# Top-k in attention: two score tiles of a pair in turn on VectorE, and the steps of three other engines laid out anew around them

## What is computed

```python
# attention: q, k, v of shape (4, 8, 576, 64)
scores = scale * np.matmul(q, k.transpose(0, 1, 3, 2))
kth = np.partition(scores, -32, axis=-1)[..., -32:-31]
scores = np.where(scores >= kth, scores, -1000000000.0)
attn = np.exp(scores - np.max(scores, axis=-1, keepdims=True))
attn = attn / (np.sum(attn, axis=-1, keepdims=True) + 1e-09)
x = np.matmul(attn, v)            # then laid out as (2304, 512)
# dense: w_in (512, 2048), w_out (2048, 512)
h = x @ w_in
x = (h * np.cos(h)) @ w_out
# experts: w_gate, w_output_gate (512, 8), w1 (8, 512, 1024), w2 (8, 1024, 512)
e = argmax(x @ w_gate)
out = softmax(x @ w_gate)[e] * sigmoid(x @ w_output_gate)[e] * (relu(x @ w1[e]) @ w2[e])
```

## Time and profile before

| what | us |
|---|---|
| median of 3 runs | 1418.0 |
| lowest and highest run | 1417.39, 1425.48 |
| profiled execution, from outside | 1417.38 |
| its span | 1415.8 |
| TensorE busy (PE) | 1266.2 (89%) |
| weight loads (PEld) | 803.3 (57%) |
| VectorE busy (DVE) | 939.5 (66%) |
| ScalarE busy (ACT) | 656.0 (46%) |
| GpSimd busy (POOL) | 562.1 (40%) |

### The profile page before, as it was taken

How to read it: one execution, slowest core, us unless ns; L and a number is a source line. 1 busy time by engine, 2 the same in 40 slices (tenths; PEclk the granted TensorE clock), 3 DMA queues, 4 the chain that set the end, 5 groups by cost and what they waited for, 6 DMA issues and landing times. The chain is left out here.

```text
span 1415.8 us, 18220 instructions
## 1 busy us (share of the span) xinstructions
PE 1266.2 (89%) x5962; PEld 803.3 (57%) x5963; DVE 939.5 (66%) x1690; ACT 656.0 (46%) x1082; POOL 562.1 (40%) x696
## 2 busy tenths in 40 slices
PE   4557899989999999899899999899399999999996
PEld 2435656856747747648658558476244444444443
DVE  6999998999999999999999999905211111111110
ACT  3455665666666766665766756624011111111110
POOL 2444463364563564654454554614411111111111
PEclk9567999999999999999999999999699999999999
DMA  8301001101001100100010000003034442243000
GB/s 245 95 8 25 1 8 33 42 8 40 1 9 41 41 8 16 25 8 16 19 47 16 1 16 1 1 16 127 24 136 150 147 150 103 73 167 128 15 13 1
DMA packets 81839, 71.52 MB, mean 51 GB/s; under 512 B 62266, under 2 KB 62266, under 8 KB 81248
## 3 DMA queue, kind: packets, MB, share of 16 engines
q1 hardware_dynamic: 76192, 60.86, 13.4%
q0 software_dynamic: 5568, 9.65, 2.2%
HBM read 62.97 MB, written 11.45 MB: 53 GB/s over the span
## 5 line engine op out<-in xcount | busy, mean ns | idle before, releaser
L720 DVE MAX8 tops<-scores_left 128x8 f32<-128x576 f32 x432 | 327.3, 758 | 12.3
L407 POOL TENSOR_TENSOR probs<-scores,probs 128x576 f32<-128x576 f32 x144 | 211.0, 1465 | 244.1 <-ACT probs L514 244.1
L976 PE MATMUL dense_banks<-x_T,weights 128*128 128x256 f32 x1024 | 246.4, 396 | 16.6 <-ACT h_T L552 16.6
L986 PE MATMUL dense_banks<-weights,h_T 128*128 128x512 f32 x512 | 236.6, 605 | 0.0
L976 PEld LDWEIGHTS dense_banks<-x_T,weights 128*128 128x128 f32 x1024 | 196.6, 197 | 58.0 <-ACT h_T L552 20.0
L723 DVE MATCH_REPLACE8 scores_left<-tops,scores_left 128x576 f32<-128x576 f32 x288 | 213.9, 743 | 0.0
L1128 PE MATMUL dense_banks<-weights,expert_h_T 128*128 x400 | 183.8, 592 | 0.0
L1109 PE MATMUL score_banks<-weights,x_gathered_T 128*128 x400 | 182.1, 598 | 1.0 <-DVE x_gathered_T L864 1.0
L514 ACT ACTIVATE probs<-scores,top_consts 128x576 f32<-128x576 f32 x144 | 111.5, 775 | 120.9 <-POOL top_consts L404 120.7
L986 PEld LDWEIGHTS dense_banks<-weights,h_T 128*128 128x128 f32 x512 | 93.4, 193 | 106.9 <-issue 106.9
L869 DVE COPY expert_h_T<-dense_banks 128x512 f32<-128x512 f32 x25 | 17.3, 692 | 185.5 <-PE dense_banks L1119 185.5
(11 more groups left out here) (160 smaller groups left out, 1581.3 us busy)
## 6 DMA issues: line engine op xcount, KB each, us to landing
weights<-in_moe_w SPq DMA_DIRECT2D x16, 2048.0 KB, 10.8
y_rows<-y_rows_sb SPq DMA_DIRECT2D x18, 256.0 KB, 2.0
k_rows<-in_k SPq DMA_DIRECT2D x32, 128.0 KB, 2.7
q_rows<-in_q SPq DMA_DIRECT2D x16, 256.0 KB, 3.4
v_rows<-in_v SPq DMA_DIRECT2D x32, 128.0 KB, 2.3
weights<-in_moe_w_in SPq DMA_DIRECT2D x1, 4096.0 KB, 13.0
weights<-in_moe_w_out SPq DMA_DIRECT2D x1, 4096.0 KB, 22.4
k_rows<-in_k SPq DMA_DIRECT2D x16, 32.0 KB, 2.6
```

The lines of the kernel that those rows point to most:

```text
L407: nc.gpsimd.tensor_tensor(ex, SS[:, u % 3, i, :], ex, ALU.subtract).then_inc(s["masked_done"], 1)
L720: V.max(top, src).then_inc(s["tops_done"], 1)
L976: last = MM(HO[:, f % 2, 0:BT], win[:, kd, f * P:(f + 1) * P], XT[:, m % 2, kd, :], start=kd == 0, stop=kd == KD - 1)
L986: last = MM(HO[:, t, :], HS[:, f, t * P:(t + 1) * P], wout[:, f, :], start=f == 0, stop=f == NF - 1)
```

## The change

On VectorE the two tiles of a pair take turns: first MAX8 of tile 0, first MAX8 of tile 1, first replacement of tile 0, and so on, seven operations each. WK has a buffer for each tile. An operation waits for the previous one of its own tile, by the count of tops_done that tops_at gives. VectorE now takes pair st in step st; the order of its pairs stays the same. The reciprocals of pair st - 2 stand behind the third operation, and the two parts of reduce_h behind the second and the third.

On GpSimd one instruction makes the constants of both tiles; a step is: constants of st - 1, denominators of st - 2, both masks of st - 1, the two products with the reciprocals for st - 2, and then all four pieces of the gate. On ScalarE a step is: copy_scores(st), both exps of st - 2, two copies of h, both below of st - 1, copy_probs(st - 3), both parts of the sine, two copies of h, copy_y, copy_x, the small copies, absolute. In TensorE's outputs the wait is for two f instead of four.

```diff
--- before.py
+++ after.py
@@ -122,6 +122,11 @@
 SMALL = small_bank_order()
 N_SMALL = len(SMALL)
 MOE_FILLS = NF + BLOCK
+
+
+def tops_at(u, i, op):
+
+    return 14 * u + 2 * op + i + 1
 
 
 def y_fill(t):
@@ -208,7 +213,7 @@
         VE = sb("v_rows", [P, HP, KB, 2 * D], stack=att)
         VR = sb("v_left", [P, HP, 2 * D], stack=att)
         SS = sb("scores", [P, 3, 2, S], stack=att)
-        WK = sb("scores_left", [P, S], stack=att)
+        WK = sb("scores_left", [P, 2, S], stack=att)
         TOP = sb("tops", [P, 3, 2, TOPK], stack=att)
         TC = sb("top_consts", [P, 3, 2, 2], stack=att)
         EX = sb("probs", [P, 3, 2 * S], stack=att)
@@ -396,15 +401,28 @@
             pool.wait_ge(s["const_ready"], n_const[0])
             pool.dma_start(table.rearrange("(p s) w -> p s w", p=P), table_init[:]).then_inc(s["table_written"], 16)
 
+            def consts(u):
+                pool.wait_ge(s["tops_done"], tops_at(u, 1, 6))
+                at_least(pool, s["exps_done"], 2 * (u - 2))
+                nc.gpsimd.tensor_tensor(TC[:, u % 3, :, :], TOP[:, u % 3, :, 0:TOPK:TOPK - 1],
+                                        factors[:].unsqueeze(1).to_broadcast([P, 2, 2]), ALU.mult).then_inc(s["consts_done"], 1)
+
             def mask(u, i):
 
-                a = u % 3
-                pool.wait_ge(s["tops_done"], (2 * u + i) * 7 + 7)
-                at_least(pool, s["exps_done"], 2 * (u - 3) + i + 1)
-                nc.gpsimd.tensor_tensor(TC[:, a, i, :], TOP[:, a, i, 0:TOPK:TOPK - 1], factors[:], ALU.mult).then_inc(s["consts_done"], 1)
                 pool.wait_ge(s["below_done"], 2 * u + i + 1)
-                ex = EX[:, a, i * S:(i + 1) * S]
+                ex = EX[:, u % 3, i * S:(i + 1) * S]
                 nc.gpsimd.tensor_tensor(ex, SS[:, u % 3, i, :], ex, ALU.subtract).then_inc(s["masked_done"], 1)
+
+            def denominators(u):
+                pool.wait_ge(s["exps_done"], 2 * u + 2)
+                at_least(pool, s["rden_done"], u - 1)
+                nc.gpsimd.tensor_scalar_add(DEN2[:, u % 2, :], DEN[:, u % 3, :], 1e-9).then_inc(s["den_done"], 1)
+
+            def normalise(u):
+                pool.wait_ge(s["rden_done"], u + 1)
+                for i in range(2):
+                    nc.gpsimd.tensor_scalar(EX[:, u % 3, i * S:(i + 1) * S], EX[:, u % 3, i * S:(i + 1) * S], RD[:, u % 2, i:i + 1], 1.0,
+                                            ALU.mult, ALU.mult).then_inc(s["probs_ready"], 1)
 
             def gate(st, piece):
 
@@ -417,24 +435,17 @@
                                                 ALU.mult).then_inc(s["gated_done"], 1)
 
             for st in range(LOOP):
-                u = st - 2
-                if 0 <= u < NS:
-                    mask(u, 1)
-                gate(st, 0)
-                if 0 <= u < NS:
-                    pool.wait_ge(s["exps_done"], 2 * u + 2)
-                    at_least(pool, s["rden_done"], u - 1)
-                    nc.gpsimd.tensor_scalar_add(DEN2[:, u % 2, :], DEN[:, u % 3, :], 1e-9).then_inc(s["den_done"], 1)
-                gate(st, 1)
+                if 0 <= st - 1 < NS:
+                    consts(st - 1)
+                if 0 <= st - 2 < NS:
+                    denominators(st - 2)
                 if 0 <= st - 1 < NS:
                     mask(st - 1, 0)
-                gate(st, 2)
-                if 0 <= u < NS:
-                    pool.wait_ge(s["rden_done"], u + 1)
-                    for i in range(2):
-                        nc.gpsimd.tensor_scalar(EX[:, u % 3, i * S:(i + 1) * S], EX[:, u % 3, i * S:(i + 1) * S], RD[:, u % 2, i:i + 1], 1.0,
-                                                ALU.mult, ALU.mult).then_inc(s["probs_ready"], 1)
-                gate(st, 3)
+                    mask(st - 1, 1)
+                if 0 <= st - 2 < NS:
+                    normalise(st - 2)
+                for piece in range(4):
+                    gate(st, piece)
 
             for t in LAST:
                 for f in range(0, NF, 4):
@@ -509,7 +520,7 @@
 
             def below(u, i):
                 a = u % 3
-                act.wait_ge(s["consts_done"], 2 * u + i + 1)
+                act.wait_ge(s["consts_done"], u + 1)
                 at_least(act, s["probsT_done"], u - 2)
                 nc.scalar.activation(EX[:, a, i * S:(i + 1) * S], SS[:, u % 3, i, :], ACT.Relu, bias=TC[:, a, i, 1:2],
                                      scale=-BIG).then_inc(s["below_done"], 1)
@@ -611,14 +622,10 @@
             for st in range(LOOP):
                 u = st - LAG
                 dense = block_at(st)
-                if 0 <= st - 2 < NS:
-                    below(st - 2, 1)
                 if st < NS:
                     copy_scores(st)
-                for m, i in dense:
-                    if i in (3, 5):
-                        sine(m, (i - 3) // 2, 1)
                 if 0 <= st - 2 < NS:
+                    exps(st - 2, 0)
                     exps(st - 2, 1)
                 for m, i in dense:
                     if i < 4:
@@ -626,16 +633,15 @@
                         copy_h(m, 4 * i + 1)
                 if 0 <= st - 1 < NS:
                     below(st - 1, 0)
+                    below(st - 1, 1)
                 if 0 <= u < NS:
                     copy_probs(u)
-                if 0 <= st - 1 < NS:
-                    exps(st - 1, 0)
                 for m, i in dense:
+                    if i in (3, 5):
+                        for h in range(2):
+                            sine(m, (i - 3) // 2, h)
                     if i < 4:
                         copy_h(m, 4 * i + 2)
-                    if i in (2, 4):
-                        absolute(m, (i - 2) // 2)
-                    if i < 4:
                         copy_h(m, 4 * i + 3)
                     if i in (6, 7):
                         copy_y(2 * m + i - 6)
@@ -655,7 +661,7 @@
                     copy_keys(b, p)
                 for m, i in dense:
                     if i in (2, 4):
-                        sine(m, (i - 2) // 2, 0)
+                        absolute(m, (i - 2) // 2)
                 if st >= LOOP - 2:
                     late_copy(LAST[0], st - (LOOP - 2))
 
@@ -707,48 +713,49 @@
         def _(dve):
             V = nc.vector
 
-            def top_k(u, i):
-                done = (2 * u + i) * 7
-                src = SS[:, u % 3, i, :]
-                if i == 0:
-                    dve.wait_ge(s["scores_copied"], u + 1)
-                at_least(dve, s["consts_done"], 2 * (u - 3) + i + 1)
-                for rnd in range(TOPK // 8):
-                    if i == 1 and rnd == 2 and u >= 1:
-                        reciprocals(u - 1)
-                    top = TOP[:, u % 3, i, rnd * 8:rnd * 8 + 8]
+            def top_op(u, i, op):
+
+                rnd = op // 2
+                top = TOP[:, u % 3, i, rnd * 8:rnd * 8 + 8]
+                src = SS[:, u % 3, i, :] if op < 2 else WK[:, i, :]
+                if op == 0:
+                    if i == 0:
+                        dve.wait_ge(s["scores_copied"], u + 1)
+                    at_least(dve, s["consts_done"], u - 2)
+                else:
+                    dve.wait_ge(s["tops_done"], tops_at(u, i, op - 1))
+                if op % 2 == 0:
                     V.max(top, src).then_inc(s["tops_done"], 1)
-                    dve.wait_ge(s["tops_done"], done + 2 * rnd + 1)
-                    if rnd < TOPK // 8 - 1:
-                        V.match_replace(WK[:], top, src, NEG).then_inc(s["tops_done"], 1)
-                        dve.wait_ge(s["tops_done"], done + 2 * rnd + 2)
-                        src = WK[:]
+                else:
+                    V.match_replace(WK[:, i, :], top, src, NEG).then_inc(s["tops_done"], 1)
 
             def reciprocals(u):
                 dve.wait_ge(s["den_done"], u + 1)
                 at_least(dve, s["probs_ready"], 2 * (u - 1))
                 V.reciprocal(RD[:, u % 2, :], DEN2[:, u % 2, :]).then_inc(s["rden_done"], 1)
 
-            def reduce_h(m, g):
-                dve.wait_ge(s["dense_emptied"], m * MOE_FILLS + 8 * (g + 1))
-                at_least(dve, s["gated_done"], (2 * (m - 1) + g + 1) * 4)
+            def reduce_h(m, g, part):
                 hs = HS[:, g * 8:(g + 1) * 8, :].rearrange("p a n -> p (a n)")
                 r1 = R[:, g, :, :].rearrange("p a n -> p (a n)")
-                V.tensor_scalar(r1.bitcast(I32), hs, 1.0 / TWO_PI, None, ALU.mult).then_inc(s["reduced_done"], 1)
-                dve.wait_ge(s["reduced_done"], m * 4 + 2 * g + 1)
-                V.scalar_tensor_tensor(out=r1, in0=r1.bitcast(I32), scalar=-TWO_PI, in1=hs,
-                                       op0=ALU.mult, op1=ALU.add).then_inc(s["reduced_done"], 1)
+                if part == 0:
+                    dve.wait_ge(s["dense_emptied"], m * MOE_FILLS + 8 * (g + 1))
+                    at_least(dve, s["gated_done"], (2 * (m - 1) + g + 1) * 4)
```

(26 more changed lines are left out.)

## The result

| what | before | after |
|---|---|---|
| median, us | 1419.31 | 1360.65 |
| lowest and highest run, us | 1417.39, 1425.48 | 1359.01, 1361.44 |
| span of the profiled execution, us | 1415.8 | 1358.9 |
| VectorE busy, us | 939.5 | 851.5 |
| TensorE busy, us | 1266.2 | 1245.0 |

The ratio is 0.9579, with an interval of 0.9556 to 0.9602: 58.7 us faster. The prediction was 1363 us.

What follows compares the result with a forecast made beforehand. VectorE was taken to set the pace, with TensorE close behind. Gains of 11 us in the first pairs, 40 in the dense steps and 3 at the end made 54, from 1417.4 to 1363 us; range 1332 to 1404.

Steps and rivals of the forecast that it cites:

- The early start: On VectorE, an instruction not held by the one in front starts 0.12 us earlier, 1.65 us a pair, giving 9.9 us.
- The first part: First ten pairs, before dense work, where VectorE alone counts: step 11 starts at about 117.4 us, 11 us gained.
- the hand-over: A pair's way through four engines, put at 9 to 10 us in the first ten steps; decides from 9.9 us on.
- The dense steps: Step 11 to the loop's end: TensorE takes over as the bound, 776 us becomes 736, 40 us gained.
- floor: TensorE's least time for the dense steps, between 700 and 723 us, taken as 711.
- pauses: TensorE's stalls and waits for h and GpSimd's products, with the clock behind them: 3.3 us a block, 25 us in all.
- rival D: TensorE's pauses vanish and the floor is reached: 91 us gained, 1326 us; chance 0.09.
- The end: Step 72: the values' 3.83 us wait for the probabilities' copy shrinks, 3 us gained; what follows is unchanged.
- A: No earlier start behind a MAX8, VectorE stays the bound at 11.56 us a pair: 1422 us; chance 0.12.
- B: Slower: the loop through four engines becomes the bound, 1479 us, or about 1435 in some steps only; chance 0.08.
- C: TensorE's pauses are worse than counted, 6 us a block instead of 3.3: 1384 us; chance 0.13.

Runs made afterwards that it cites:

- e1: Changed kernel, but VectorE sorts tile 0 to the end and then tile 1, the rest of the new plan kept: 1406.14 us, 0.9956 of the kernel before.
- e2: Changed kernel with tiles in turn, but every VectorE operation waits for the one directly in front: 1428.95 us, 1.0109 of the kernel before.
- a0: The changed kernel itself once more, nothing altered: 1358.99 us, 0.9574 of the kernel before.
- e4: Changed kernel with one search round less on VectorE (24th largest value as limit, so another result): 1320.19 us, 0.9342 of the kernel before.
- e8: Changed kernel with the reciprocals behind the second part of the reduction of h instead of in front: 1345.57 us, 0.9519 of the kernel before.
- e9: Changed kernel with two GpSimd products ahead of the normalisations and the reciprocals behind the reduction's second part: 1346.25 us, 0.9482 of the kernel before.
- e10: Kernel before with turns and two scores_left buffers, reciprocals behind the sixth operation of the pair after next: 1405.09 us, 0.9887 of the kernel before.
- e11: Changed kernel with each tile's constants in an instruction of its own, below waiting for its tile alone: 1359.25 us, 0.9568 of the kernel before.
- e3: Kernel before with only the turns and two scores_left buffers, reciprocals behind twelve operations of the next pair: 1411.08 us, 0.9991 of the kernel before.
- e6: Changed kernel with the sines back at their old places on ScalarE: 1414.24 us, 1.0007 of the kernel before.
- e5: Changed kernel with TensorE's outputs waiting for the gated pieces of four f at once, as before: 1363.27 us, 0.9651 of the kernel before.
- e7: Changed kernel with two of GpSimd's four products in front of the two normalisations: 1347.67 us, 0.9542 of the kernel before.

## Why the prediction was right, term by term

TensorE's and VectorE's rows of the changed kernel, both ends of the dense steps, against the earlier trace rows:

```profile
98.36 2.29 PE L933 MATMUL score_banks<-k_T,q_T 64*128 64x288 f32 x8
...
108.36 2.29 PE L933 MATMUL score_banks<-k_T,q_T 64*128 64x288 f32 x8
...
119.40 2.19 PE L933 MATMUL score_banks<-k_T,q_T 64*128 64x288 f32 x8
...
843.95 3.70 PE L994 MATMUL dense_banks<-weights,h_T 128*128 128x512 f32 x8
...
853.75 0.49 PE L969 MATMUL small_banks<-probs_T,v_left 128*128 128x128 f32 x2 [1.69 <-ACT probs_T L547]
...
857.61 5.90 PE L994 MATMUL dense_banks<-weights,h_T 128*128 128x512 f32 x8 [2.34 <-POOL h_T L434]
...
869.10 1.16 PE L1037 MATMUL score_banks<-x_T,weights 128*128 128x128 f32 x8
```

**The early start** was put at 0.12 us, with 0.13 as a bound. It is 0.13 to 0.14: a pair takes 9.7 us, not 9.9.

The Trainium skill ("VectorE: DVE Perf Modes", "The DRAIN you can't avoid") says that a chain of eight copies was no faster with one semaphore than with eight; the MAX8 of e1 and e2 do not agree, 0.67 to 0.68 us without the wait for the instruction in front and 0.80 with it. The same section of the Trainium skill also says that a next operation that is not held starts earlier; the prediction left that out, and with it e1 and e2 agree.

**The first part**, predicted 11 us: step 11 starts at 119.40 instead of 128.68, 9.3 us. From the seventh pair on the hand-over was the limit, as these rows of TensorE (98.36, 108.36) and this one of VectorE say:

```profile
101.85 1.42 DVE L728 MAX8 tops<-scores 128x8 f32<-128x576 f32 x2 [0.20 <-ACT scores L539]
```

The prediction had the loop at "9 to 10" in the slow clock and the decision at 9.9, and let VectorE win. It was 10.0. In a0, where the loop did not bind, step 11 starts at 116.89, 0.5 us from the predicted 117.4.

**The dense steps**, predicted 40 us: from 119.40 to 843.95 it is 724.5 us instead of 776.2, 51.6 us gained. Busy times of this stretch, before and after:

```profile
128.68:904.85 776.17, 724.33 (x4013) 508.92 (x4012) 735.28 (x1310) 512.63 (x856) 402.11 (x485) 0.97 0.08 19
```

```profile
119.40:843.95 724.55, 701.08 (x4013) 497.69 (x4012) 659.33 (x1306) 501.20 (x855) 395.70 (x425) 1.00 0.08 21
```

The same 4013 MATMULs are busy 23 us less, at the full clock, and TensorE's idle time falls from 51.8 to 23.5 us. The prediction had 711 us of floor, the middle of 700 to 723 for want of a view of how much time the slow clock took, and 25 us of pauses. With the busy time as the floor, the mis-sized term is the floor, 10 us too high, and the pauses were 1.5 too large. Measured by e4, which still has 7.1 us of waits of its own in its 705.1, the miss is 6 us of floor and 6 of pauses (19.4). The clock came back whole (0.97 to 1.00), where the twelve pauses for the products last 1.6 us at most. So rival D, which counted with the floor and no pauses, was half true.

Inside the pauses one term was too small as well: the reduction was put at 1.3 and 2.6 us, as in the earlier trace rows, and takes 1.6 and 2.9 on average, 3.48 for the second part in each block's first half, because of GpSimd beside it (e8).

**The end**, predicted 3 us: 904.85 - 843.95 = 60.9 us ahead at step 72, 63.0 at the values (853.75), so 2.1 of the 3. Then the outputs of step 73 wait 2.34 us for the products and run in slow clock (5.90 us), and at the first late tile it is 60.1 (929.22 against 869.10). That pause was not in the sum at this place. Behind it the changed kernel loses another 3 us before the routing, in two waits of ScalarE whose releaser lies outside the engines of the core; TensorE waits 7.2 us there, 4.3 in the kernel before. The same 7.2 us stand in a0, e9, e10 and e11, and 0.7 in all of e1 to e8, so they go with the chip and not with the change: e10 has the old plan and has them too. What is waited for stays open.

Together 9.3 + 51.6 - 0.8 - 3.2 = 56.9 us in the profiled executions. The total was right to 3 us because one term was 12 us too small and the three others together 9 us too large (the first part by 2, the end by 4, and 3 behind it, put at nothing). The mechanism was right; that the sum came so close is partly luck.

**Rivals.** A fell with e1 and e2. B as a whole fell, but it ruled from the seventh pair to step 11, and e3, e6 and e10, with the same early starts and 46 to 60 us slower than the changed kernel, suggest how near it was behind that. C was put at 6 us a block; the 23.5 us of idle time are 3.1 us a block.

## What to carry to other kernels

When one engine runs a chain of short operations, put another chain's operation between each two: a start is early when the thing waited for is not the instruction directly in front, and at 576 elements that is 0.13 us of 0.8. Before counting on it, lay out the whole round that the engine hands to the others and gets back, because the gain ends where that round is longer than the engine's new period; here turns without the new plan brought nothing, or 16 us at best, and the plan without the turns 6 us at best. Then look at what the release of one engine lets start on another: moving a 0.15 us reciprocal behind a reduction gave 6 to 8 us. And slack at the start of an engine's round is not slack at its end: follow the result onward, too, before calling the engine's time free.

## What the hardware showed that was not expected

GpSimd and VectorE slow each other, and not evenly. Where GpSimd's two normalisations run beside the second part of VectorE's reduction, they take 3.42 to 3.51 us instead of 1.46; the reduction takes 3.48 us instead of 2.27 in the first half of each block (149.11) and stays at 2.27 to 2.40 in the second (174.11). In e8 it is GpSimd's two masks that run beside it: they take 5.17 us instead of 2.79 (145.37), and the reduction stays at 2.27 (147.00). Which of them loses was not looked into further.

In the first ten steps the clock moves between its two levels in some executions (scores in 1.24 to 1.97 us) and stays at or next to 1.2 GHz in others (2.18 to 2.29 us). Two executions of the changed kernel start step 11 at 119.40 and 116.89 us, 2.5 us apart, with no other difference found in front of it. The others fall in line: e5, e7 and e8, where it moved, start it at 116.89 to 117.30 us, e9 and e11, where it did not, at 119.56 and 118.93.
